# Preparing the next expert's weights in three groups instead of two, with a relu between the first two

## What is computed

```python
do_compute = x @ w_skip > 0                    # about half of the 3072 tokens
xc = x[do_compute]
e_idx = argmax(xc @ w_gate, axis=1)            # one of 8 experts for each token
for e in range(8):
    h = maximum(xc[e_idx == e] @ w1[e], 0)     # 512 -> 1024
    y[e_idx == e] = gate * (h @ w2[e])         # 1024 -> 512
out[do_compute] = xc + y
```

## Time and profile before

| | |
|---|---|
| time, median of 3 runs | 936.69 us (936.14 to 938.19) |
| the profiled execution | 938.59 us, span 937.1 us |
| PE busy | 914.0 us, 98% of the span |
| DVE / ACT / POOL busy | 472.6 / 420.8 / 81.7 us |
| chain that ended last | PE 91%, issue 2%, ACT 2%, DVE 2%, DMA 1% |
| `w_hi` copies (L775), `w_lo` subtractions (L1457) | 70 each, 1050 and 1220 ns |
| HBM read / written | 77.72 / 25.56 MB |

### The profile page before, as it was taken

How to read it: one execution, slowest core, us unless ns; L and a number is a source line. 1 busy time by engine, 2 the same in 40 slices (tenths; PEclk the granted TensorE clock), 3 DMA queues, 4 the chain that set the end, 5 groups by cost and what they waited for, 6 DMA issues and landing times.

```text
span 937.1 us, 16992 instructions
## 1 busy us (share of the span) xinstructions
PE 914.0 (98%) x5152; PEld 731.1 (78%) x5153; DVE 472.6 (50%) x1419; ACT 420.8 (45%) x970; POOL 81.7 (9%) x147
## 2 busy tenths in 40 slices
PE   7999999989999998999999999999999999999998
PEld 5778777767888876788888887888888888878886
DVE  5787899876666767653242234222422332242224
ACT  7888999844666667542131223111311222232122
POOL 3111111123111111100000000000000000000000
PEclk9999999989999999999999999999999999999999
DMA  5556774375666688620021003000400040004001
GB/s 197 168 164 218 222 239 152 98 282 187 233 243 225 234 309 301 234 46 1 0 63 28 1 1 85 4 0 0 90 0 0 0 90 0 0 0 90 0 0 45
DMA packets 87364, 99.52 MB, mean 106 GB/s; under 512 B 56093, under 2 KB 56221, under 8 KB 87312
## 3 DMA queue, kind: packets, MB, share of 16 engines
q1 hardware_dynamic: 81168, 83.34, 28.3%
q0 software_dynamic: 6000, 15.49, 4.9%
q10 hardware_dynamic: 144, 0.07, 0.0%
HBM read 77.72 MB, written 25.56 MB: 110 GB/s over the span
## 4 chain that ended last, share of the span: by engine, by line
PE 91%; issue 2%; ACT 2%; DVE 2%; DMA 1%; ACTq 1%; DVEq 0%; SPq 0%
PE bank L1128 29%; PE bank L1114 29%; PE bank L1029 7%; PE bank L1010 7%; PE bank L869 5%; PE bank L924 4%; PE bank L897 4%; PE bank L935 1%; PE bank L1018 1%; PE bank L949 1%; PE bank L917 1%; DMA w_raw<-in_weights 1%; PE bank L1002 1%; ACT prob L667 0%; DVE x_row L1304 0%
## 5 line engine op out<-in xcount | busy, mean ns | idle before, releaser
L1498 DVE TENSOR_TENSOR g<-relu_c 128x512 f32<-128x512 f32 x96 | 66.4, 692 | 353.9 <-ACT relu_c L812 353.8
L812 ACT ACTIVATE relu_c<-bank 128x512 f32<-128x512 f32 x96 | 57.3, 597 | 385.1 <-PE bank L1114 385.1
L1114 PE MATMUL bank<-x_hi,w_lo 128*128 128x512 f32 x384 | 151.5, 395 | 0.7 <-DVE x_lo L1485 0.7
L1128 PE MATMUL bank<-w_hi,g_lo 128*128 128x512 f32 x384 | 152.0, 396 | 0.0
L1128 PE MATMUL bank<-w_lo,g_hi 128*128 128x512 f32 x384 | 151.7, 395 | 0.0
L1114 PE MATMUL bank<-x_lo,w_hi 128*128 128x512 f32 x384 | 151.6, 395 | 0.0
L1128 PE MATMUL bank<-w_hi,g_hi 128*128 128x512 f32 x384 | 151.5, 395 | 0.0
L1114 PE MATMUL bank<-x_hi,w_hi 128*128 128x512 f32 x384 | 151.5, 395 | 0.0
L667 ACT ACTIVATE prob<-score,neg_max 128x264 f32<-128x264 f32 (+1 forms) x192 | 94.0, 496 | 15.0 <-DVE neg_max L1190 15.0
L1457 DVE TENSOR_TENSOR w_lo<-w_raw,w_hi x70 | 81.9, 1220 | 21.3 <-ACT w_hi L775 10.3
L1128 PEld LDWEIGHTS bank<-w_hi,g_lo 128*128 128x128 f32 x384 | 72.1, 188 | 18.8 <-DVE g_lo L1505 1.6
(11 more groups left out here) (149 smaller groups left out, 1282.1 us busy)
## 6 DMA issues: line engine op xcount, KB each, us to landing
w_raw<-in_weights SPq DMA_DIRECT2D x80, 512.0 KB, 5.0
k_in<-in_kT SPq DMA_DIRECT2D x24, 264.0 KB
q_in<-in_qT SPq DMA_DIRECT2D x24, 256.0 KB, 3.4
v_in<-in_v SPq DMA_DIRECT2D x24, 256.0 KB
x_rows<-x_row SPq DMA_DIRECT2D x24, 256.0 KB
x_row<-x_rows SPq DMA_DIRECT2D x96, 64.0 KB, 2.4
out<-w_raw SPq DMA_DIRECT2D x12, 512.0 KB, 2.9
x_res<-routed POOLq DMA_DIRECT2D x15, 260.0 KB, 3.3
```

Of the source, the lines that this page charges most:

```text
L1114: ins = eng.matmul(hc_ps[f % 2][:, :], w[f // UNIT][:, f % UNIT, wcols], x[:, c, :], start=(c == 0 and n == 0), stop=(c == DC - 1 and n == 2))
L1128: ins = eng.matmul(yc_ps[s][:, :], gg[:, f % 2, s * P:(s + 1) * P], w[f // UNIT][:, f % UNIT, DM:CH], start=(f == 0 and n == 0), stop=(f = ...
L1498: eng.tensor_tensor(g[:, f % 2, :], relu_c[:, f % 2, :], relu_c[:, f % 2, :], ALU.mult).then_inc(s_cg, 1)
```

## The change

The first group is split. `GROUPS` gives for each group its first chunk, its size in a first tile, and the chunk that is made again in a later tile: chunks 0 and 1, chunks 2 and 3, chunks 4 to 7; made again are 3, 3 and 7. ACT's order becomes `chunks(0)`, `relu_b(n, 0)`, `chunks(1)`, `h_upper(n, 0)`, and so on; DVE's becomes `chunks(0)`, `chunks(1)`, `h_lower(n, 0)`, and so on. The landings of chunks 0 and 1 count on `s_whead`, those of chunks 2 and 3 on the new `s_wmid`. PE's and POOL's code is the same, SP's differs in the semaphore of two chunks.

```diff
+GROUPS = ((0, 2, HEAD - 1), (2, 2, HEAD - 1), (HEAD, UNIT - HEAD, UNIT - 1))
...
             if f == 0:
-                nc.scalar.wait_ge(s_whead, 16 * HEAD * u)
+                nc.scalar.wait_ge(s_whead, 16 * 2 * u)
+            elif f == 2:
+                nc.scalar.wait_ge(s_wmid, 16 * (HEAD - 2) * u)
...
         def parts_ahead(e, n, later=0):
-            return e * (UNIT - 2) + n * 2 + later * (UNIT - 2) + UNIT
+            return e * (UNIT - len(GROUPS)) + n * len(GROUPS) + later * (UNIT - len(GROUPS)) + UNIT
...
+        def made_ahead(e, n, k, later):
+            return later * (UNIT - len(GROUPS) - GROUPS[k][0] + k) + parts_ahead(e, n) + GROUPS[k][0]
...
# ACT, in chunks(k)
-                    before_is_later = is_later(eng, n, first + 1) if k == 0 else 0
-                    lower = parts_ahead(e, n) + later * (UNIT - 2)
-                    eng.wait_ge(s_wlo, lower if k == 1 else lower - (UNIT - HEAD) + before_is_later * (UNIT - HEAD - 1))
+                    if k == 0:
+                        before_is_later = is_later(eng, n, first + 1)
+                        eng.wait_ge(s_wlo, later * (UNIT - len(GROUPS)) + before_is_later * (UNIT - HEAD - 1) + parts_ahead(e, n) - (UNIT - HEAD))
+                    elif k == 1:
+                        eng.wait_ge(s_wlo, later * (UNIT - HEAD + UNIT - len(GROUPS) + 1) + parts_ahead(e, n) - (UNIT - HEAD))
+                    else:
+                        eng.wait_ge(s_wlo, later * (UNIT - len(GROUPS)) + parts_ahead(e, n))
...
                 chunks(0)
                 relu_b(n, 0)
+                chunks(1)
                 h_upper(n, 0)
                 relu_b(n, 1)
                 x_upper(n + 1)
                 h_upper(n, 1)
                 eng.wait_ge(s_by, n + 1)
-                chunks(1)
+                chunks(2)
...
# DVE
                 chunks(0)
+                chunks(1)
                 h_lower(n, 0)
                 x_lower(n + 1)
                 h_lower(n, 1)
-                chunks(1)
+                chunks(2)
                 take_y(n)
```

More of the change, by code:

```diff
@@ L350, in parts_ahead @@
         def parts_ahead(e, n, later=0):
-            return e * (UNIT - 2) + n * 2 + later * (UNIT - 2) + UNIT
+            return e * (UNIT - len(GROUPS)) + n * len(GROUPS) + later * (UNIT - len(GROUPS)) + UNIT
         def group(k, later):
-            first, size = ((0, HEAD), (HEAD, UNIT - HEAD))[k]
-            return size - later * (size - 1), later * (size - 1) + first
+            first, size, remade = GROUPS[k]
+            return size - later * (size - 1), later * (remade - first) + first
+        def made_ahead(e, n, k, later):
+            return later * (UNIT - len(GROUPS) - GROUPS[k][0] + k) + parts_ahead(e, n) + GROUPS[k][0]
         def is_later(eng, n, first):
@@ L425, in load_chunk @@
             def load_chunk(u, f):
-                eng.dma_start(w_raw[:, f, :], weights[u, :, f, :]).then_inc(s_whead if f < HEAD else s_wtail, 16)
+                eng.dma_start(w_raw[:, f, :], weights[u, :, f, :]).then_inc(s_whead if f < 2 else s_wmid if f < HEAD else s_wtail, 16)
             load_q(0)
@@ L763, in chunks @@
                     size, shift = group(k, later)
-                    made = parts_ahead(e, n) + (later * (UNIT - 2) if k == 0 else later * (UNIT - HEAD - 1) + HEAD)
+                    made = made_ahead(e, n, k, later)
                     eng.wait_ge(s_whi, made)
                     close(eng)
-                    before_is_later = is_later(eng, n, first + 1) if k == 0 else 0
-                    lower = parts_ahead(e, n) + later * (UNIT - 2)
-                    eng.wait_ge(s_wlo, lower if k == 1 else lower - (UNIT - HEAD) + before_is_later * (UNIT - HEAD - 1))
+                    if k == 0:
[5 more added lines that the diff above has]
+                        eng.wait_ge(s_wlo, later * (UNIT - len(GROUPS)) + parts_ahead(e, n))
                     close(eng)
-                    chunk_loaded(e + 1, k * HEAD)
+                    chunk_loaded(e + 1, GROUPS[k][0])
                     with eng.Fori(0, size) as c:
```

2 lines of the change are left out of this document (1 added, 1 removed).

## The result

The changed kernel takes 940.15 us (median of 20 runs, 939.14 to 942.71) against 937.03 for the kernel before on the same chips: 3.1 us between the medians; the ratio over all runs is 1.0031, 95% interval 1.0023 to 1.0040, which is 2.9 us. The forecast was slower by 5.2: 941.9, with a range of 937.0 to 945.0. The profiled execution took 941.0, its span is 939.5.

The account below looks back on a forecast made before the run. PE was taken as the bound, so only its waits in the expert layer count: 3.2 + 1.6 + 3.4 + 1.5 - 4.5 = +5.2 on the median 936.69 gave 941.9 us, range 937.0 to 945.0.

Parts of the forecast that it names:

- the likeliest case: The whole forecast with the clock falling in tile 1: 941.9 us, chance 0.50.
- rival 1: The clock holds in tile 1, all else as forecast: +3.6, 940.3 us; chance 0.20.
- Tile 1: Expert 0's second tile: PE pauses 3.2 at layer 2 for h_upper, plus 1.6 for a clock fall.
- Second tiles: Second tiles of experts 1 to 4: h_upper late behind the same-tile subtraction wait, 0.85 new stall each, 3.4 together.
- now 0.72 later, 277.93: Expert 2's second tile: DVE's subtraction, which ended at 277.21, moves by 0.72 to 277.93.
- DVE's pause between groups: DVE waits for its own first group before chunks(1): 0.72 in every tile, bounds 0 and 1.0.
- Rival 2: DVE's pause between groups is covered: -2.2 to -0.6, about 935.3 us; chance 0.09.
- The chain of experts 5 to 7: Tiles of the one-tile experts and expert 7's first: of 6.1 lost to relu stalls, 4.5 is gained.
- DVE has become the bound there: Experts 5 to 7: DVE's h_lower comes 0.2 then 1.2 late, so the gain is 4.5, not 6.1.
- Expert 7's second tile: DVE behind by its chain, so h_upper ends at 381.3, wanted at 379.8: 1.5 of stall.
- The relu would be on time: Expert 6: relu due at 350.15 is on time if the first two loads have landed by 348.1.
- `h_upper(0)` in first tiles: h_upper behind two copies ends at 6.1 against 6.27, in time by 0.15: costs nothing, upper bound 2 in all.

Follow-up runs that it names:

- The first kernel: Changed kernel, but later tiles make chunks 1 and 2 again instead of chunk 3 twice, so ACT needs no same-tile subtraction: 936.55 us, ratio to before 0.9993.
- The ninth: Changed kernel with ACT's relu_b(n, 0) put back behind both head groups: 960.96 us, ratio to the kernel before 1.027.
- the eighth kernel: Changed kernel with the first four loads on one semaphore again, ACT's first group waiting for all four: 941.33 us, ratio to the kernel before 1.0041.
- Kernel six: Kernel before the change, with spare DVE reductions whose result nothing reads, put just before h_lower(n, 1): 943.54 us, ratio 1.0066.
- the seventh: Kernel before the change, with spare DVE reductions whose result nothing reads, put behind h_lower(n, 1): 937.25 us, ratio 1.0011.

## Why the prediction was right, and where its sizes were off

The measured 940.15 lies inside the range, and just below the likeliest case's own range of 940.3 to 943.5. It is nearest to rival 1's 940.3, although the clock did fall in the profiled execution; the sizes below say how.

**The order of the argument held.** PE was the bound, and only waits at the seams of ACT and DVE counted. The change removed the two relu stalls and put one wait in their place, for the subtraction of the same tile. The first kernel shows this is the cause and not the seven more chunks: with as many chunks and no such wait, all of the layer 2 stalls are gone. The ninth shows it from the other side.

**Tile 1: 4.8 forecast, 5.25 measured.** The pause was 3.37 for 3.2, the clock about 1.5 for 1.6. Rival 1, the clock holding, did not happen in the profiled execution, but did in the eighth kernel after a pause of 2.83. So it may go either way from one execution to the next, and the sum for one execution is uncertain by 1.5.

**Second tiles: 3.4 forecast, 2.14 measured.** The step "now 0.72 later, 277.93" was mis-sized, and so was "alike". The subtraction was forecast to end 5.06 into each of these tiles; it ended at 4.48, 4.86, 4.75 and 5.20 in experts 1 to 4, and the tiles are 0.2, 0.6, 0.5 and 0.9 longer, in the same order. `h_upper` also started 0.97 after the copy did instead of 1.05. The terms 0.36 (0.37 measured) and 0.72 (0.73, below) were right.

**DVE's pause between groups: right.** DVE's timeline in expert 5's tile, 340.90 to 354.24, of the kernel after:

```profile
344.23 2.36 DVE L1469 TENSOR_TENSOR w_lo<-w_raw,w_hi  x2 [2.13 <-issue]
347.33 2.36 DVE L1469 TENSOR_TENSOR w_lo<-w_raw,w_hi  x2 [0.73 <-DVE w_lo L1469]
...
350.81 0.68 DVE L1423 TENSOR_TENSOR hb_lo<-bank,hb_hi 128x512 fp32r<-128x512 f32 x1
351.40 4.62 DVE L1469 TENSOR_TENSOR w_lo<-w_raw,w_hi  x4
```

This decides between the row and the Trainium skill's page "VectorE: DVE Perf Modes", section "The DRAIN you can't avoid", by which a semaphore behind each operation costs nothing extra: within a group that holds (two in 2.36), and a wait with register work behind it costs 0.73. Rival 2, the side on which the change would have been faster, rested on this pause being covered, and it was not.

**The chain of experts 5 to 7: -4.5 forecast, -4.44 measured, by another way.** The sum was right, the places were not: that they add up to the forecast is luck. The forecast let PE wait for `hb_lo` (1.4 in expert 7's first tile); no such wait is in the trace. `h_lower(n, 1)` of expert 5 ended at 351.49, 10.59 into the tile and earlier than PE wanted it, and PE lost 0.83 at the next expert's first matmul, and 0.52 at the one after. Expert 5's tile, which the forecast left at 12.67, became 13.34; expert 6's became 13.16 and not 12.6, expert 7's first 12.48 and not 13.7. The step "DVE has become the bound there" is right; the step that a late operand costs only what it is late at its own matmul is wrong. Kernel six against seven shows this, and so does the constant 2.75.

**Expert 7's second tile: 1.5 forecast, 0.46 measured,** for the same reason: PE had been held at two boundaries, so DVE was less far behind it. The subtraction began 3.54 into the tile (383.42) where the forecast had 4.5, and the pause at 386.62 is 0.23.

**The two loads.** "The relu would be on time" came true in expert 6, but not thanks to the split semaphore: in the eighth kernel that tile is the same with a wait for all four. The relu in front of two copies was enough, together with loads that were ready sooner by PE's clock: ACT could begin 1.31 into the tile there, against 2.84 in the kernel before. The split was worth 1.4 in the tile behind it.

**`h_upper(0)` in first tiles** cost nothing, as forecast, and the margin was as worked out: in the first tiles of experts 1 to 7 it ended 0.18 or 0.19 before PE's matmul began, which less the 0.05 of release is 0.13 for the 0.15 forecast.

All in all 1.3 too much in second tiles, 1.0 too much in expert 7's last, 0.4 too little in tile 1: +5.2 becomes 3.3, and the measurement says 2.9 to 3.1.

## What to carry to other kernels

When one loop body serves a long and a short case, read the short one for dependences that the long one doesn't have: two groups that make the same chunk turned a buffer that was free a tile ago into one that is free 5 us into this tile. Whatever is queued behind such a wait decides its price: from the same wait it was 3 us for the kernel and 24 with the relu behind it, and with other chunks made again, so without the wait, the time was that of the kernel before. And when an edit holds or reorders loads, follow the queue to its end: the best version here (0.42% faster than before) needed a load of another layer moved ahead.

## What the runs showed of the hardware

**An operand that is in time for its matmul can still be late for the engine's sequencer.** Between experts PE's queue has register work (reading the next expert's bounds). Where `hb_lo` is early, no idle time shows there (tiles of 12.34), so this work is hidden behind matmuls. In the sixth kernel, an `hb_lo` that was ready at 10.9 into the tile, about 0.5 before its matmul, cost 0.47 to 1.16 at five of the boundaries, and in the seventh the same work elsewhere cost none. At the boundary of experts 5 and 6 PE's next matmul came 2.75 to 2.77 after `h_lower(n, 1)` ended, in nine traces. The reading that the sequencer stops at the matmul whose operand is open, and so starts the register work too late, fits all of these; the sequencer's position itself was not measured.

**The length of a pause does not say whether the clock falls.** In the ninth kernel a pause of 2.31 left it at 1.00, and one of 1.98 was followed by 0.50. PE's timeline and the rows by 1 us:

```profile
345.51 0.66 PE L1030 MATMUL bank<-ident,h_b 128*128 128x128 f32 x4 [2.31 <-ACT h_b L744]
...
387.42 0.66 PE L1030 MATMUL bank<-ident,h_b 128*128 128x128 f32 x4 [1.98 <-ACT h_b L744]
```

```profile
346.00:347.00 1.00, 1.00 (x7) 0.82 (x6) 0.81 (x2) 0.60 (x1) 0.00 (x0) 1.00 0.79 262
...
388.00:389.00 1.00, 1.00 (x5) 0.76 (x4) 0.53 (x1) 0.60 (x1) 0.00 (x0) 0.64 0.85 271
389.00:390.00 1.00, 1.00 (x4) 0.75 (x3) 1.00 (x2) 0.00 (x0) 0.00 (x0) 0.50 0.87 293
```

Across kernels it is the same: the clock was at 0.50 after 2.29 in the sixth (at 372.94) and 2.50 in the seventh (at 352.98), and at 1.00 after 2.29 in the ninth (at 290.15) and 2.83 in the eighth.

The Trainium skill, page "TensorE: Matmul & The Clock Gate", section "What's actually happening", says that the monitor runs free of the kernel's events; these six pauses agree with it, and do not prove it.
